# Opening re-ordered: conversions first, two loads ahead of the bulk of the weights, values and weights a step later

## What is computed

```python
keep = is_sink | in_window
scores = np.where(keep, scale * (q @ k.T), -1e9)
a = softmax(scores); attn = a @ v
x = attn as (3072 tokens, 512)
h = x @ w_in                       # 512 x 2048
x2 = (h - tanh(h)) @ w_out         # 2048 x 512
logits = x2 @ w_gate + modality_bias[modality_id]
# top-1 of 8 experts, gate weight from the softmax:
out = gate_w * (relu(x2 @ w1[e]) @ w2[e])
```

## Time and profile before

| | |
|---|---|
| median of 3 runs | 1072.42 us |
| the profiled execution | 1070.08 us, span 1068.1 us |
| busy share of the span | TensorE 93%, DVE 61%, ScalarE 54%, GpSimd 31% |
| mean granted TensorE clock | 0.981 of full speed |
| chain that ended last | TensorE 73%, DVE 12%, ScalarE 6%, issue 5% |
| median landing after issue | queries and keys 3.4 us, values 7.0 us, w_in part 9.6 us, w_out part 9.0 us |

### The profile page before, as it was taken

The page is one execution under the profiler, slowest core; times in us unless marked ns, Lnnn a source line. Parts: engine busy times, 40 slices in busy tenths (PEclk is TensorE's granted clock), DMA queues, the critical chain, the costliest instruction groups (busy, mean ns, idle before and its releaser), DMA issues.

```text
span 1068.1 us, 23850 instructions
## 1 busy us (share of the span) xinstructions
PE 989.9 (93%) x7968; PEld 605.0 (57%) x7968; DVE 650.4 (61%) x2272; ACT 581.4 (54%) x1329; POOL 327.3 (31%) x462
## 2 busy tenths in 40 slices
PE   2748999999999999999999999999899999899996
PEld 1524444555554555555455556555487777677774
DVE  6665767667768767777866775646765334633331
ACT  4766786666667765766666675536422224522221
POOL 5766675112116211213511210101032232232322
PEclk9958999999999999999999999999999999999999
DMA  8710001201100320100210010041024211111111
GB/s 315 256 36 19 18 19 66 79 19 35 48 18 19 64 79 19 49 18 19 37 48 19 19 48 1 2 159 59 1 51 174 75 49 54 40 41 49 49 47 40
DMA packets 24375, 60.30 MB, mean 56 GB/s; under 512 B 9504, under 2 KB 9760, under 8 KB 22752
## 3 DMA queue, kind: packets, MB, share of 16 engines
q1 hardware_dynamic: 15392, 45.77, 13.2%
q0 software_dynamic: 5728, 13.43, 4.0%
q10 hardware_dynamic: 3168, 0.02, 0.1%
HBM read 45.35 MB, written 14.12 MB: 56 GB/s over the span
## 4 chain that ended last, share of the span: by engine, by line
PE 73%; DVE 12%; ACT 6%; issue 5%; POOL 1%; DVEq 1%; DMA 1%; ACTq 0%; SPq 0%; POOLq 0%
PE h_ps L751 19%; PE acc L807 18%; PE h_ps L1907 5%; PE s_ps L1856 5%; PE pt_ps L1856 5%; PE acc L1907 5%; PE pt_ps L639 4%; PE s_ps L569 3%; PE x_out L706 3%; ACT probs L587 2%; PE s_ps L858 1%; DVE qk_top L401 1%; PE pt_ps L662 1%; DVE pt_lo L648 1%; PE x_out L1833 1%
## 5 line engine op out<-in xcount | busy, mean ns | idle before, releaser
L807 PE MATMUL acc<-w_out_all,g_hi 128*128 128x512 f16 x768 | 228.4, 379 | 0.0
L751 PE MATMUL h_ps<-xt_hi,w_in_all 128*128 128x384 f16 x960 | 196.8, 328 | 4.2 <-DVE g_raw L772 3.0
L807 PE MATMUL acc<-w_out_all,g_lo 128*128 128x512 f16 x384 | 146.0, 380 | 3.3 <-DVE g_lo L792 2.7
L751 PEld LDWEIGHTS h_ps<-xt_hi,w_in_all 128*128 128x128 f16 x960 | 91.3, 100 | 62.3 <-issue 7.4
L807 PEld LDWEIGHTS acc<-w_out_all,g_hi 128*128 128x128 f16 x768 | 75.1, 98 | 77.7
L763 ACT ACTIVATE g_raw<-h_ps,batch_scale 128x384 f32<-128x384 f32 x120 | 69.5, 579 | 89.2 <-PE h_ps L751 85.3
L792 DVE SCALAR_TENSOR_TENSOR g_lo<-g_raw,batch_scale,g_hi 128x384 f16<-128x384 f32 x128 | 84.6, 661 | 44.4 <-ACT g_hi L782 44.4
L782 ACT ACTIVATE g_hi<-g_raw,batch_scale 128x384 f16<-128x384 f32 x128 | 77.9, 608 | 55.4 <-DVE g_raw L772 54.0
L101 POOL TENSOR_TENSOR tick<-tick 1x1 f32<-1x1 f32 x83 | 15.6, 188 | 293.4 <-ACT y L1923 116.2
L580 DVE CUSTOM_DVE_ANT_0 probs<-s_ps,mask 128x260 f32<-128x260 f32 (+1 forms) x192 | 70.0, 402 | 49.7 <-issue 43.9
L751 PE MATMUL h_ps<-xt_lo,w_in_all 128*128 128x384 f16 x480 | 98.3, 328 | 0.0
(11 more groups left out here) (315 smaller groups left out, 2098.2 us busy)
## 6 DMA issues: line engine op xcount, KB each, us to landing
qk_raw<-in_qk SPq DMA_DIRECT2D x31, 454.0 KB, 3.4
raw<-in_w SPq DMA_DIRECT2D x16, 512.0 KB, 8.1
v_raw<-in_v SPq DMA_DIRECT2D x4, 1536.0 KB, 7.0
x_tokens<-x SPq DMA_DIRECT2D x24, 256.0 KB, 2.5
w_in_all<-in_w_in SPq DMA_DIRECT2D x4, 1024.0 KB, 9.6
w_out_all<-in_w_out SPq DMA_DIRECT2D x4, 1024.0 KB, 9.0
x_tokens<-g_raw SPq DMA_DIRECT2D x1, 1024.0 KB, 12.7
vs_raw<-in_v SPq DMA_DIRECT2D x24, 4.0 KB
```

What stands on the lines that cost most here:

```text
L751: mm = eng.matmul(h_of(m, f), w16[0][:, f, x * DM + k * P:x * DM + (k + 1) * P], r[:, par, k, :], start=(i == 0), stop=(i == 3 * KD - 1))
L807: mm = eng.matmul(acc[t][:, :], l[f % 2][:, t * P:(t + 1) * P], w16[1][:, f, x * DM:(x + 1) * DM], start=(f == 0 and i == 0), stop=(f == N ...
```

## The change

`conversions` moves ahead of `prepare_alone` in each half step. Group 1's two conversions stand both in half step 2, group 2's maxima in 5 and its conversions in 7, and those of groups 3 to 5 a half step or so earlier than before. The value maxima are dealt out as one, three and two; value scale, multiplies and splits, the sinks and all weight steps stand later (the last three value blocks in half steps 13 to 21). Pair 1's and pair 2's value products stand both in step 4. In the queue of loads group 3 goes ahead of the last two parts of w_in, and group 4 ahead of the last three parts of w_out; the turn g = 4 of `loads` keeps its value load. `sink_halves` waits for the three value splits in place of a conversion. One more tile of w_in is split in the first window, seven instead of six.

```diff
--- before.py
+++ after.py
@@ -524,7 +524,7 @@
                 eng.activation(vs_all[s][:], vs_raw[:], ACT.Copy).then_inc(q["vs_hi_done"], 1)
             if E == "pool":
                 if b == 0:
-                    eng.wait_ge(q["conv_lo"], 3)
+                    eng.wait_ge(q["v_lo_done"], TPC)
                 if b:
                     eng.wait_ge(q["qk_mult"], 2 * (2 * HP * b + 1))
                 eng.wait_ge(q["vs_hi_done"], b + 1)
@@ -1116,9 +1116,10 @@
                 load_qk(E, eng, 2)
                 load_weights(E, eng, 0, range(2))
                 load_sinks(E, eng, 0)
+                load_qk(E, eng, 3)
                 load_weights(E, eng, 0, range(2, 4))
                 load_weights(E, eng, 1, range(1))
-                load_qk(E, eng, 3)
+                load_qk(E, eng, 4)
                 load_weights(E, eng, 1, range(1, 4))
                 late_constants(E, eng)
             constants(E, eng)
@@ -1135,8 +1136,10 @@
         def conversions(E, eng, i):
 
             for g in range(1, HP * NC):
-                tops = (1, 1, 1) if g == 1 else (6 * g - 9, 6 * g - 7, 6 * g - 7)
-                splits = (2, 3) if g == 1 else (6 * g - 5, 6 * g - 3)
+                early = {1: (1, 1, 2, 2), 2: (5, 5, 7, 7)}
+                q_top, k_top, q_split, k_split = early.get(
+                    g, (6 * g - 9, 6 * g - 7) + ((6 * g - 6, 6 * g - 5) if g <= 5 else (6 * g - 5, 6 * g - 3)))
+                tops, splits = (q_top, k_top, k_top), (q_split, k_split)
                 at = divmod(g, HP)
                 for part in range(2):
                     if i == tops[part]:
@@ -1150,43 +1153,45 @@
 
         def prepare_alone(E, eng, i):
 
-            if i in (0, 2, 3):
-                v_tops(E, eng, 0, (0, 2, 3).index(i) * 2)
-                v_tops(E, eng, 0, (0, 2, 3).index(i) * 2 + 1)
-            if i == 3:
-                if E in ("dve", "pe"):
-                    spread(E, eng, 0)
+            for blk in {0: (0,), 2: (1, 2, 3), 4: (4, 5)}.get(i, ()):
+                v_tops(E, eng, 0, blk)
+            if i == 4 and E == "dve":
+                spread(E, eng, 0)
+            if i == 5 and E == "pe":
+                spread(E, eng, 0)
+            if i == 6:
                 v_scales(E, eng, 0)
                 for blk in range(TPC):
                     v_multiply(E, eng, 0, blk)
-            if i == 4:
+                sink_multiply(E, eng, 0)
+            if i == 7:
                 for blk in range(TPC):
                     v_split(E, eng, 0, blk)
-                sink_multiply(E, eng, 0)
-            if i == 5:
                 sink_halves(E, eng, 0)
-            if i in (4, 5, 6, 7):
-                weight_gram(E, eng, 0, i - 4)
-            if i in (6, 8, 10):
-                v_multiply(E, eng, 0, i // 2)
-            if i in (7, 9, 11):
-                v_split(E, eng, 0, (i - 1) // 2)
-            if i == 8:
+            if i in (6, 7, 8, 9):
+                weight_gram(E, eng, 0, i - 6)
+            if i in (13, 17, 20):
+                v_multiply(E, eng, 0, TPC + (13, 17, 20).index(i))
+            if i in (14, 18, 21):
+                v_split(E, eng, 0, TPC + (14, 18, 21).index(i))
+            if i == 10:
                 weight_diagonal(E, eng, 0)
-            if i == 9:
+            if i == 12:
                 weight_scale(E, eng, 0)
-            if i in (10, 11, 13, 14, 15, 16, 20, 22, 25, 26):
-                weight_split(E, eng, 0, (10, 11, 13, 14, 15, 16, 20, 22, 25, 26).index(i))
-            if i in (10, 11, 13, 15):
-                weight_gram(E, eng, 1, (10, 11, 13, 15).index(i))
+            w_in_at = (13, 14, 15, 16, 18, 20, 22, 24, 26)
+            if i in w_in_at:
+                weight_split(E, eng, 0, w_in_at.index(i))
+            if i in (11, 12, 13, 15):
+                weight_gram(E, eng, 1, (11, 12, 13, 15).index(i))
             if i == 16:
                 weight_diagonal(E, eng, 1)
-            if i == 17:
+            if i == 18:
                 weight_scale(E, eng, 1)
-            if i == 18:
+            if i == 19:
                 batch_scales(E, eng, 0)
-            if i in (18, 19, 23, 24):
-                weight_split(E, eng, 1, (18, 19, 23, 24).index(i))
+            w_out_at = (19, 21, 23, 25)
+            if i in w_out_at:
+                weight_split(E, eng, 1, w_out_at.index(i))
             if i == 26:
                 if E == "dve":
                     late_constants(E, eng)
@@ -1194,8 +1199,9 @@
         def prepare(E, eng, w, k):
 
             if w == 0:
-                if k in (1, 3, 5, 8, 11, 17):
-                    weight_split(E, eng, 0, 10 + (1, 3, 5, 8, 11, 17).index(k))
+                w_in_at = (0, 1, 3, 5, 8, 11, 17)
+                if k in w_in_at:
+                    weight_split(E, eng, 0, NF - 7 + w_in_at.index(k))
                 if k in (0, 2, 4, 6, 7, 12, 15, 19, 21, 23, 27, 28):
                     weight_split(E, eng, 1, 4 + (0, 2, 4, 6, 7, 12, 15, 19, 21, 23, 27, 28).index(k))
                 if k == SLOTS - 2:
@@ -1238,7 +1244,8 @@
                     stage(transpose_probs, E, eng, r - 1)
                     if r + 1 < ALONE:
                         score_pair(E, eng, r + 1)
-                    stage(weigh_values, E, eng, r - 2)
+                    for of in {3: (), 4: (1, 2)}.get(r, (r - 2,)):
+                        stage(weigh_values, E, eng, of)
                 if E == "act":
                     score_pair(E, eng, r)
                     stage(transpose_probs, E, eng, r - 1)
@@ -1252,16 +1259,16 @@
                         score_pair(E, eng, r + 1)
                     stage(split_x, E, eng, r - 2)
                     stage(transpose_sinks, E, eng, r - 1)
+                conversions(E, eng, 2 * r)
                 prepare_alone(E, eng, 2 * r)
-                conversions(E, eng, 2 * r)
                 if E == "pe":
-                    if r in (4, 8):
+                    if r in (5, 8):
                         weight_spread(E, eng, r // 8)
                     stage(transpose_sinks, E, eng, r - 1)
                 if E == "act":
                     stage(transpose_sinks, E, eng, r - 1)
+                conversions(E, eng, 2 * r + 1)
                 prepare_alone(E, eng, 2 * r + 1)
-                conversions(E, eng, 2 * r + 1)
 
         scored = {2 * (r - ALONE): r for r in range(ALONE)}
 
@@ -1336,7 +1343,8 @@
         def loads(eng):
 
             for g in range(4, HP * NC):
-                load_qk("sp", eng, g)
+                if g > 4:
+                    load_qk("sp", eng, g)
                 if g % (2 * HP) == HP and g // (2 * HP) + 1 < B:
                     load_v("sp", eng, g // (2 * HP) + 1)
                     load_sinks("sp", eng, g // (2 * HP) + 1)
```

## The result

The changed kernel takes 1083.94 us, the median of four runs (1083.22 to 1084.56); before, in the same session, 1072.45. The ratio is 1.0109, interval 1.0095 to 1.0123: 1.1% slower, 11.5 us. 1083 was predicted.

What follows compares the result with a forecast made beforehand. The opening, where attention works alone and engines other than TensorE set the pace, was taken to decide: +2.8 us without DVE's wait, +11.7 with it, giving 1081.8 from the profiled 1070.08 or 1084.1 on the median; predicted 1083, range 1075 to 1090.

Steps and rivals of the forecast that it cites:

- The stall: Half step 21: DVE waits 10.6 us for group 5's load, queued behind values issued only after the last value split.
- whether group 5 is held by the values ahead of it: Group 5 lands behind the values at 83.8 us; with 3.4 us from issue it would be there at 82.2.
- part 1: First conversions and values: an early 6 us gain is lost to the later value scale; pair 5 masked 3.1 us late.
- part 2: Weight scales behind sink transposes: pair 8 masked 5.7 us late, pair 10 1.3 late, its exponentials 4.05 us late.
- +4.05 us at pair 10: ScalarE waits for the second weight's scale and starts pair 10's exponentials at 69.7 us instead of 65.65.
- only the stall: Rival: ScalarE reaches pair 10 when it does now, leaving DVE's wait for group 5: +7.6 us, 1078; chance 0.21.
- The sum: First hidden product at 95.9 us instead of 84.24: +11.7 us, or +2.8 without DVE's wait for group 5.
- part 3: Loads of groups 3 and 4 ahead of weight parts, delaying those parts: cost 0.
- The term for slot 0 of the first window: One weight split moves from the opening to the first window's slot 0: taken as 0, bounds -0.5 and +1.5.
- no wait: Rival: the load queue isn't held, so DVE doesn't wait at group 5: +2.8 us, 1074 to 1075; chance 0.06.
- faster: Rival: the early 6 us gain lasts, with later key waits some 10 us in all: about 1062; chance 0.07.
- A colder TensorE: Rival: TensorE stays at the low clock to 60 us after idling from about 29.6: +4 to +5, 1087; chance 0.14.

Runs made afterwards that it cites:

- run 1: Changed kernel with the next batch's values and sinks issued behind group 5's load instead of ahead of it: 1075.48 us, ratio 1.0028.
- run 2: Kernel before with only the last three value blocks moved, multiplied in half steps 13, 17, 20 and split in 14, 18, 21: 1082.73 us, ratio 1.009.
- run 3: Changed kernel, load queue untouched, last two value blocks multiplied in half steps 15 and 17 and split in 16 and 18: 1077.2 us, ratio 1.004.
- Run 4: Run 1's kernel with the value scale, its multiplies and the sink multiply in half step 5 instead of 6: 1072.77 us, ratio 0.9996.
- run 9: Kernel before with the weights' part of the change alone (products, scales and splits in the change's half steps): 1075.68 us, ratio 1.0024.
- run 5: Run 4's kernel with the first four w_in splits and the first w_out split one half step later: 1072.8 us, ratio 0.9999.
- run 10: Kernel before with the values' part of the change alone, group 5's load ahead of the next batch's values: 1079.21 us, ratio 1.0055.
- run 7: Kernel before with the conversions' part of the change alone (ahead of `prepare_alone`, new table of half steps): 1069.07 us, ratio 0.9964.
- run 6: Run 5's kernel with group 2's two conversions in half step 8 instead of 7, behind the three value splits: 1071.74 us, ratio 0.9992.

## Why the prediction was right

**The stall.** The decisive step, that SyncE's turn g = 4 holds group 5 behind values that are split in the same half step in which DVE needs group 5, holds in all its parts. Predicted and measured: last value split 76.25 and 76.37; group 5 issued 78.9 and 78.97; there at 83.8 and 84.4; DVE's arrival 73.2 and 73.1; its wait 10.6 and 11.3. Runs 1, 2 and 3 take the stall away, make it alone, and shorten it by moving the deadline. The one doubt of that part, whether group 5 is held by the values ahead of it, falls out for holding: 5.4, 5.4 and 5.6 us from issue in the changed kernel and runs 2 and 3, 1.4 to 2.1 us behind the values, and 3.4 us in run 1, where no values are ahead of it. The rule of the Trainium skill cited there ("DMA: Bandwidth & Descriptors", "Queues, rings and completion order") is that each DMA engine consumes the descriptors of a queue in ring order. The traces agree with it, since the group landed behind the values each time. The rule speaks of consuming and not of landing, though, and landing times don't rule out that the two loads only shared the engines' rate.

**The values (part 1).** Pair 3's scores predicted near 18.2, measured 18.65; three blocks split by 36.7, measured 36.75; pair 5 masked at 38.7, measured 38.61. Run 4 bears out the cause: the scale 3.3 us earlier brings pair 5 2.3 us earlier and the time back by 0.3%.

**The weights (part 2).** ScalarE's first split of w_in predicted to end at 53.4; it started at 53.21 and so ended 0.5 us late. Pair 8 masked at 55.4, measured 55.58; pair 10 masked at 64.4, measured 64.43; exponentials of pair 10 predicted at 69.7, measured 69.96. As a cause of the time the part holds alone (run 9, +0.24%), but within the changed kernel it isn't additive: run 5 takes both waits away and gains nothing. Of the 2.0 us that its pair 13 is early, 1.5 are gone at the first hidden product, and in between stands the 1.42 us wait for GpSimd. The prediction's +4.05 us at pair 10 was right as a time in the trace; to read it as the part of the sum that goes when the waits go, as the rival "only the stall" did, would have been wrong.

**The sum.** The first hidden product was predicted at 95.9 and came at 96.75, 12.5 late instead of 11.7; by medians the kernel is 11.5 us later. Of the 0.85 us by which the list is short, 0.6 are group 5's landing (84.39 for 83.8) and 0.3 the stretch from there to the first hidden product (12.36 for 12.1). Behind it come the 2.0 us of the tail, which the sum had at 0, so that the profiled execution took 1084.56 where its sum gave 1081.8. That the median fits to 1 us is partly luck: the sum started from an execution 2.3 us below its kernel's median. The clock behind the first hidden product was taken as unchanged; over ten us it was 0.85 against 0.77 before, so it added nothing to the lateness. The loads (part 3) cost nothing that shows: TensorE waits for no DMA in the changed trace. No run tries their new order by itself. The term for slot 0 of the first window was taken as 0, and the 950 us behind the first hidden product show no cost there. Of the rivals, "no wait" and "faster" fell with the 11.3 us wait. "A colder TensorE" had something: 16 products of w_out's sum at 45.69 took 1.91 us, at the low clock, where 1.08 had been put in. It didn't last: pairs 8 and 10 are masked within 0.2 us of the list, and DVE stands ready for group 5 at 73.08, where the list had 73.2:

```profile
45.69 1.91 PE L295 MATMUL acc<-w_out_all 128*128 128x128 bf16 x16
```

By ratios, on the kernel before: conversions -0.36%, weights +0.24%, values +0.55% (with the loads in order), the stall +0.8% (run 1 against the changed kernel) or +0.9% (run 2). The first three add to +0.4%, run 1 measures +0.28% for all of them together; early conversions take away waits for keys that weights and values alone keep (14.6 us up to 100 us in run 9, 12.6 in run 10, 1.2 in the changed kernel).

## What to carry to other kernels

When work is moved in a kernel whose engines run written lists, look for whoever waits on that work's count, in the load queue above all: a release that comes later holds every load behind it, even one whose own buffer has long been free. A stall taken away from one engine's list often shows up in the next one; run 7's gain doubled only when ScalarE's in-order wait for the sinks was moved as well. And a first product that comes earlier in one trace is not a kernel that ends earlier, until the clock there and the medians have been compared.

## What the runs showed of the hardware

TensorE's granted clock goes from 0.50 to 1.00 at different distances from the first hidden product, with the same products behind it: about 3 us in run 5's kernel, about 9 us in run 6's and run 9's. In all three TensorE works for some 4 us, stands 1.6 us for DVE (L772) and works on; in run 5's the clock rose ahead of that wait, in the other two only behind it. Twenty us from the first hidden product hold a mean clock of 0.92, 0.77 and 0.76. From there to the end run 5's execution takes 986.1 us and run 6's 988.7: 2.6 us between two executions, as much as several of the edits tried here.

What decides it wasn't found. TensorE had been at the low clock for 20 us before in run 5's kernel and for 25 in run 6's; in run 9's it had been up for a part of the ten us before (0.76 and 0.58 over two stretches of five). In the last 5 us it had 2.62 us of work in all three. It need not be a matter of the kernel: these are single executions, those of runs 6 and 9 the slowest of their ten, and the unchanged kernel before itself took from 1070.25 us (mean clock 0.981) to 1075.21 (0.975) in the 25 executions beside runs 1, 2, 4 and 7.
